# Pooling two batches of v sooner, and spreading the last stage's loads, in a pooled-attention, MLP and mixture-of-experts kernel

## The chip, the cores and the metric

The kernel runs on one core of a Trainium2 chip. The metric is the device time of one execution in microseconds. Before the change three runs took 1186.99, 1190.72 and 1192.93 us, so the median is 1190.72 us.

## The reference

```python
k_p = k.reshape(B, H, Sp, pool, D).mean(axis=3)      # B = H = 8, S = 576, D = 64, pool = 8
v_p = v.reshape(B, H, Sp, pool, D).mean(axis=3)
attn = softmax(scale * q @ k_p.T)
x = (attn @ v_p)  -> (4608, 512)
h = (x @ w1) * (x @ w2) @ w3
y = h @ w_out                                        # d_ff = 1024
logits = y @ w_gate + modality_bias[modality_id]     # 8 experts, top 1
out = gate * (relu(y[mask] @ e_w1[e]) @ e_w2[e])     # per expert
```

Everything is float32. The kernel gets that precision from reduced-precision matmuls by splitting each operand into a high and a low part (`xh` and `xl`, `wh` and `wl`) and running three matmuls for one product: the lines 726, 727 and 728, all in the helper `split`.

## The kernel before, in words

The work falls into a weight stage, nine stages for attention and the first MLP product, a stretch for the second product and the routing, and a loop over expert tiles. Each engine has one instruction queue written out by hand. The engines meet only at semaphores, and an instruction that waits holds up everything behind it on its engine. The same holds for the queues of DMA instructions: SyncE (SP) issues the loads of k, v, x and the weights, ScalarE (ACT) those of q and all stores of `g_rows`.

**Stages.** Stage b (0 to 7) multiplies 512 tokens of batch b by w1 and w2. The 64 tokens of each batch that are left over are collected in DRAM (`left_x`) and make stage 8. A stage has four positions i (`first_position` for stage 0, `position` for the others), and a position has seven products n. Products (`product(b, i, n)`, 12 matmuls each) are the seven block products of a Strassen-like scheme. They rotate through three PSUM banks, shown as `ab`, `x2p` and `rt`. VectorE (DVE) and ACT take them out: `copy_p` (L1139) on ACT and `chain` (L1512) on DVE, which `u2`, `u3`, `u4_c22` and `c12` call in this order in each position. A product may start only once the one three before it has been taken out. At the end of a position GpSimd (POOL) multiplies the two halves: `first_quarter` (L613, L621) and `other_quarters` (L627, L633) write `gst`, and ACT stores that to `g_rows` (`store_g`, L1145, L1148, L1150). L633 may overwrite `gst` only when the stores of the position before have landed (`g_out[1]`), and `u2` of the next position waits for L633.

**Attention for the next batch** is laced into the stage before. `score(b, m)` (L805, m = 0 to 4) are the five rounds of q times pooled k for batch b, all in one pair of PSUM banks `sct`. So each round waits for `sub_done`, which `soft_max` on DVE (L1459, L1461) gives once it has read the round before. `exp_p`, `norm`, `soft_sum` and `soft_turn` finish a round; `exp_p` also issues the q load (`qt`) for the round two later. `weigh_v(b, 0)` and `weigh_v(b, 1)` (L826) multiply the probabilities by pooled v (`vp4`). Then `raw_x`, `x_sum` (L1498), `hi_x` (L1128) and `lo_x` (L1504) make `xf`, `xh` and `xl` of batch b for its own stage.

**Pooling.** `pool_k(b, m)` (L572, L577) and `pool_v(b, m)` (L584, L587) sum groups of eight rows on POOL, in one of two slots `kv`. v of a batch comes in three parts. SP runs `bring_v(b)` in this order: load v 0, load v 1, store v 0, load v 2, store v 1, store v 2, load k of batch b+1 (both halves), and then `spread_v(b)`, four loads of the stored sums into `vp4`, which need all three stores. `weigh_v(b, 0)` waits for those four.

**Behind the last batch** SP loads the four pieces of `left_x` into `xf`, then the four pieces of `w34_rows` (the product w3 times w_out, 520 KB a piece), then `load_g`, which brings `g_rows` back.

`at = 4 * b + i` counts the positions through all stages. `prod_done[n]` counts how often product n has been done.

Of the kernel before, what the change touches and what calls it, by code (L numbers as in the profile page):

```python
# [15 lines left out]
B, H, S, D = 8, 8, 576, 64  # L16
# [30 lines left out]
POS = FC // 2  # L47
# [43 lines left out]
def build(nc, q, k, v, moe_w1, moe_w2, moe_w3, moe_w_out, w_out_t, modality_id, w_gate, modality_bias,  # L91
# [7 lines left out]
    with ctx:  # L99
# [40 lines left out]
        before = small("before", [P, P], BF16, 2)  # L140
# [285 lines left out]
        def _(sp):  # L426
# [63 lines left out]
            sp.wait_ge(xl_ready, BLOCKS * B)  # L490
            for part in range(2):
                for th in range(2):
                    sp.dma_start(xf[:, RAW_X[part][th], :, :],
                                 left_x[:, 2 * part:2 * part + 2, HT * th:HT * (th + 1)]).then_inc(left_in, 16)
            sp.wait_ge(pv_done, 2 * B)
            for n in range(KEPT):
                sp.wait_ge(w34_out[n], 16 * len(range(n, 2 * FC, KEPT)))
            for n in range(4):
                sp.dma_start(w34r[:, 2 * n:2 * n + 2, :], w34_rows[:, 2 * n:2 * n + 2, :]).then_inc(w34_in[n], 16)

            def load_g(t):
# [26 lines left out]
            for t in range(NG):  # L528
                b, g = t // G, t % G
# [26 lines left out]
        def _(pool):  # L556
# [23 lines left out]
            def pool_v(b, m):  # L580
                pool.wait_ge(kv_in[m % 2], 16 * (IN_SLOT[m % 2] * b + 2 + m // 2))
                t = kv[:, m % 2, 0:2 * POOL * D].rearrange("p (c s d) -> p c s d", c=2, s=POOL)
                for w in (4, 2):
                    pool.tensor_tensor(t[:, :, 0:w, :], t[:, :, 0:w, :], t[:, :, w:2 * w, :],  # L584
                                       ALU.add).then_inc(pool_done, 1)
                    pool.wait_ge(pool_done, steps.next())
                pool.tensor_tensor(kv[:, m % 2, 2 * POOL * D:].rearrange("p (c d) -> p c d", c=2), t[:, :, 0, :],  # L587
                                   t[:, :, 1, :], ALU.add).then_inc(vp_ready, 1)
# [21 lines left out]
            def first_quarter(at):  # L610

                pool.wait_ge(x_copied, 3 * at + 2)
                pool.tensor_tensor(pair(p2c[:, :, :]), pair(p2c[:, :, :]), pair(kb[:, 0, :, :]),  # L613
                                   ALU.add).then_inc(p_sums, 1)
                pool.wait_ge(p_sums, 2 * at + 1)
                if at:
                    pool.wait_ge(g_out[0], 16 * at)
                else:
                    for n in (1, 2, 3):
                        pool.wait_ge(w34_out[n], 16 * len(range(n, 2 * FC, KEPT)))  # L620
                pool.tensor_tensor(gst[:, 0, :], p2c[:, 0, :], p2c[:, 1, :], ALU.mult).then_inc(g_ready, 1)  # L621
# [18 lines left out]
            for m in range(2):  # L640
                pool_k(1, m)
            pool_v(1, 0)
            for b in range(STAGES):
                for i in range(POS):
                    first_quarter(POS * b + i)
                    if b == 0 and i < 2:
                        pool_v(1, i + 1)
                    if b and i == 0 and b + 1 < B:
                        pool_v(b + 1, 2)
                    if i == (1 if b else 2) and b + 2 < B:  # L650
                        pool_k(b + 2, 0)
                        pool_k(b + 2, 1)
                    if b and i == 2 and b + 2 < B:
                        pool_v(b + 2, 0)
                    if i == 3 and b + 2 < B:
                        if b == 0:
                            pool_v(2, 0)
                        pool_v(b + 2, 1)
                    other_quarters(POS * b + i)

# [62 lines left out]
        def _(pe):  # L723
# [75 lines left out]
            def score(b, m):  # L799
                may_score(b, m)  # L800
                for n in range(PAIRS):
                    for g in range(4):
                        for a in range(2):
                            rows = slice(D * a, D * (a + 1))
                            mm = pe.matmul(sct[Q * g:Q * (g + 1), a, KEYS * n:KEYS * (n + 1)],  # L805
                                           qt[rows, (AT * b + m) % 2, n, Q * g:Q * (g + 1)], kp[rows, n, :],
                                           start=True, stop=True)
                mm.then_inc(scored, 1)
# [59 lines left out]
                        score(2, 0)  # L868

            def position(b, i):  # L870
                late = 2 if b == 1 and i == 0 else 0
                for n in range(BLOCKS):
                    if i < 2 and n == late and b + 1 < B:
                        score(b + 1, 2 * i + 1)
                    if i < 2 and n == 4 + late and b + 1 < B:
                        score(b + 1, 2 * i + 2)
                    product(b, i, n)
                    if i == 2 and n == 0 and b + 2 < B:
                        score(b + 2, 0)
                    if i == 2 and n == 2 and b + 1 < B:  # L880
                        weigh_v(b + 1, 0)
                    if i == 2 and n == 4 and b + 1 < B:
                        weigh_v(b + 1, 1)
# [543 lines left out]
        def _(dve):  # L1427
# [324 lines left out]
            def position(b, i):  # L1752
                at = POS * b + i
                att = b + 1 < B
                if i == 0:
                    if b > 1:
                        lo_x(b, 6)
                    if att and b > 1:
                        soft_max(b + 1, 1)
                        soft_sum(b + 1, 1)  # L1760
                    u2(at)
                    if b == 1:
                        lo_x(1, 6)
                        soft_sum(2, 0)
                    u3(at)
                    if b == 1:
                        soft_max(2, 1)
                        soft_turn(2, 0)
                    if att and b > 1:
                        soft_max(b + 1, 2)  # L1770
                    u4_c22(at)
                    if b == 1:
                        soft_sum(2, 1)
                        soft_max(2, 2)
                    if att:
                        soft_sum(b + 1, 2)
                        soft_turn(b + 1, 1)
                if i == 1:
                    if att:
                        soft_max(b + 1, 3)  # L1780
                        soft_sum(b + 1, 3)
                        soft_turn(b + 1, 2)
                    u2(at)
                    u3(at)
                    if att:
                        soft_max(b + 1, 4)
                    if b == B:
                        dve.memset(acc[:, :], 0.0).then_inc(dve_done, 1)
                        dve.wait_ge(dve_done, own.next())
                        dve.memset(rb[:, 0, :], 0.0).then_inc(dve_done, 1)  # L1790
                        dve.wait_ge(dve_done, own.next())
                        route_bias(0)
                        lo_w34(0)
                    u4_c22(at)
                    if att:
                        soft_sum(b + 1, 4)
                        soft_turn(b + 1, 3)
                    if b == B:
                        lo_w34(1)
                if i == 2:  # L1800
                    if b + 2 < B:
                        soft_max(b + 2, 0)
                    if att:
                        soft_turn(b + 1, 4)
                    if b + 2 < B:
                        soft_sum(b + 2, 0)
                    u2(at)
                    u3(at)
                    if b == B:
                        lo_w34(2)  # L1810
                    u4_c22(at)
                    if b + 2 < B:
                        soft_turn(b + 2, 0)
                    if b == B:
                        lo_w34(3)
                        lo_g(0)
                    else:
                        x_sum(b + 1, 3)
                if i == 3:
                    if b < B:  # L1820
                        x_sum(b + 1, 4)
                        x_sum(b + 1, 2)
                        lo_x(b + 1, 0)
                        x_sum(b + 1, 5)
                        lo_x(b + 1, 1)
                    u2(at)
                    u3(at)
                    if b < B:
                        lo_x(b + 1, 2)
                    u4_c22(at)  # L1830
                    if b < B:
                        lo_x(b + 1, 3)
                        lo_x(b + 1, 4)
                        lo_x(b + 1, 5)
                    else:
                        lo_g(1)
                c12(at)
# [259 lines left out]
```

## Time and profile before

| | |
|---|---|
| median of three runs | 1190.72 us (1186.99 to 1192.93) |
| the profiled execution | 1193.07 us, span 1191.2 us |
| TensorE (PE) busy | 1158.5 us, 97% of the span |
| PE weight loads busy | 1088.4 us, 91% |
| DVE, ACT, POOL busy | 637.6, 397.6, 400.9 us |
| mean granted TensorE clock | 0.993 of full speed |
| a 256 KB store of `g_rows`, issue to landing, median | 3.2 us |

The span is that of the instructions; 1.9 us lie around it. PE is idle for 32.7 us in all, and only what shortens that idle time or the slow-clock stretches can shorten the run, unless matmuls are taken away.

### The profile page before, as it was taken

To read this page: it belongs to the slowest core of one execution; us is meant where nothing else is said; L and a number is where in the kernel's file an instruction comes from. 1 tells how busy PE (TensorE), PEld (TensorE's weight loads), DVE (VectorE), ACT (ScalarE), POOL (GpSimd) and SP (SyncE) were. 2 spreads that over 40 slices of the span, in tenths; PEclk is the share of its full clock that TensorE was granted. 3 is DMA by queue.
4 is the path that set the end of the run, shared out by engine and by line. 5 is a ranking of instruction groups with operands and counts; after the bars stand their busy time and mean duration, and the time that the engine had idled before them with its cause. 6 is when DMAs were issued, how large, how long until landed. Compare 5 with 4: busy or idle time off the path is not lost.

```text
span 1191.2 us, 29759 instructions
## 1 busy us (share of the span) xinstructions
PE 1158.5 (97%) x12126; PEld 1088.4 (91%) x12127; DVE 637.6 (54%) x1228; ACT 397.6 (33%) x906; POOL 400.9 (34%) x385
## 2 busy tenths in 40 slices
PE   8899889999999999999999999999999999999996
PEld 6789779999999999999999999998998999899895
DVE  0899688798888963653444557622222252222221
ACT  1575355655556541332222324111111141111110
POOL 2337766677766654550000000211211112121111
PEclk9999999999999999999999999999999999999999
DMA  9764363644736314245545555241111101111111
GB/s 348 268 172 140 107 203 83 191 136 133 203 84 193 100 43 159 72 126 140 134 137 132 133 175 176 66 184 44 46 53 35 44 26 55 44 51 46 35 47 41
DMA packets 99890, 137.12 MB, mean 115 GB/s; under 512 B 16835, under 2 KB 66115, under 8 KB 99780
## 3 DMA queue, kind: packets, MB, share of 16 engines
q1 hardware_dynamic: 40340, 78.77, 22.0%
q10 hardware_dynamic: 53040, 36.29, 10.6%
q0 software_dynamic: 6400, 20.50, 5.4%
q8 instruction: 81, 1.33, 0.5%
q14 instruction: 29, 0.24, 0.1%
HBM read 92.99 MB, written 43.06 MB: 114 GB/s over the span
## 4 chain that ended last, share of the span: by engine, by line
PE 55%; DVE 0%; POOL 0%; issue 0%; DMA 0%; ACT 0%; ACTq 0%; POOLq 0%; DVEq 0%
PE ab L727 6%; PE ab L726 6%; PE x2p L726 6%; PE ab L728 6%; PE x2p L728 6%; PE x2p L727 6%; PE rt L727 6%; PE rt L726 6%; PE rt L728 6%; PE sct L917 1%; PE ab L908 0%; DMA out<-y_out,tok_c 0%; DVE gl L1538 0%; POOL gst L633 0%; DVE kb L1512 0%
## 5 line engine op out<-in xcount | busy, mean ns | idle before, releaser
L727 PE MATMUL ab<-xtl,e1h 128*128 128x256 f32 x608 | 170.7, 281 | 0.0
L726 PE MATMUL ab<-xth,e1h 128*128 128x256 f32 x608 | 169.6, 279 | 0.0
L728 PE MATMUL ab<-xth,e1l 128*128 128x256 f32 x608 | 169.3, 278 | 0.0
L1401 ACT ACTIVATE hth<-ab 128x512 fp32r<-128x512 f32 x76 | 45.5, 598 | 333.8 <-PE ab L728 333.8
L706 POOL DMA_INDIRECT out<-y_out,tok_c x38 | 38.4, 1012 | 319.3 <-DVE y_out L2020 318.7
L1999 DVE SCALAR_TENSOR_TENSOR htl<-ab,hth 128x512 fp32r<-128x512 f32 x76 | 52.4, 691 | 156.2 <-ACT hth L1401 156.1
L727 PEld LDWEIGHTS ab<-xtl,e1h 128*128 128x128 f32 x608 | 114.5, 188 | 0.7
L726 PEld LDWEIGHTS ab<-xth,e1h 128*128 128x128 f32 x608 | 114.1, 188 | 1.0 <-issue 0.4
L728 PEld LDWEIGHTS ab<-xth,e1l 128*128 128x128 f32 x608 | 114.3, 188 | 0.0
L726 PE MATMUL x2p<-xh,wh 128*128 128x256 f32 x336 | 98.2, 292 | 5.1 <-DVE kb L1512 4.8
L1086 ACT ACTIVATE pb<-pb,rc 128x72 f32<-128x72 f32 x320 | 83.2, 347 | 59.7 <-DVE rc L1473 59.7
L726 PE MATMUL ab<-xh,wh 128*128 128x256 f32 x336 | 96.8, 288 | 1.9 <-DVE kb L1512 1.4
L726 PE MATMUL rt<-xh,wh 128*128 128x256 f32 x336 | 97.3, 290 | 0.7 <-DVE kb L1512 0.6
L727 PE MATMUL x2p<-xl,wh 128*128 128x256 f32 x336 | 95.4, 284 | 0.0
L727 PE MATMUL rt<-xl,wh 128*128 128x256 f32 x336 | 95.2, 283 | 0.0
L727 PE MATMUL ab<-xl,wh 128*128 128x256 f32 x336 | 94.7, 282 | 0.0
L728 PE MATMUL x2p<-xh,wl 128*128 128x256 f32 x336 | 94.4, 281 | 0.0
L728 PE MATMUL rt<-xh,wl 128*128 128x256 f32 x336 | 94.1, 280 | 0.0
L728 PE MATMUL ab<-xh,wl 128*128 128x256 f32 x336 | 93.7, 279 | 0.0
L1538 DVE TENSOR_TENSOR gl<-gr,gh 128x1024 fp32r<-128x1024 f32 x36 | 45.2, 1256 | 78.4 <-ACT gh L1159 78.4
L633 POOL TENSOR_TENSOR gst<-kb 128x768 f32<-128x768 f32 x36 | 72.2, 2004 | 41.8 <-DVE kb L1512 33.2
L726 PE MATMUL x2p<-w34h,gh 128*128 128x260 f32 x288 | 82.1, 285 | 0.0
(229 smaller groups left out, 3344.8 us busy)
## 6 DMA issues: line engine op xcount, KB each, us to landing
gr<-g_rows SPq DMA_DIRECT2D x36, 512.0 KB, 4.3
kv<-in_v SPq DMA_DIRECT2D x24, 512.0 KB, 4.6
qt<-in_q ACTq DMA_DIRECT2D x38, 256.0 KB, 3.2
kv<-in_k SPq DMA_DIRECT2D x16, 576.0 KB, 5.3
g_rows<-gst ACTq DMA_DIRECT2D x72, 128.0 KB, 2.6
g_rows<-gst ACTq DMA_DIRECT2D x36, 256.0 KB, 3.2
x_rows<-xr SPq DMA_DIRECT2D x36, 256.0 KB, 3.7
stage<-in_moe_w SPq DMA_DIRECT2D x8, 1024.0 KB, 8.5
```

Source lines behind the costliest of these rows:

```text
L633: pool.tensor_tensor(gst[:, 1:4, :], kb[:, 1:4, 0, :], kb[:, 1:4, 1, :], ALU.mult).then_inc(g_ready, 1)
L706: pool.indirect_dma_start(out=out, out_offset=bass.IndirectOffsetOnAxis(ap=tok_c[:, n:n + 1], axis=0), in_=y_out[:, half, :], in_offset=No ...
L726: pe.matmul(outp, lh, rh, start=first, stop=False)
L727: pe.matmul(outp, lh, rl, start=False, stop=False)
L728: return pe.matmul(outp, ll, rh, start=False, stop=last)
L917: mm = pe.transpose(bank[:, n, :], xg[:, 2 * r + half, n * P:(n + 1) * P], ident[:, :])
L1086: ins = act.activation(p, p, ACT.Copy, scale=rc[r % 2][:, h:h + 1])
L1401: act.activation(hth[:, 2 * n:2 * n + 2, :].rearrange("p f n -> p (f n)"), ab[n // 2][:, n % 2, :], ACT.Relu).then_inc(hth_ready, 1)
L1538: dve.tensor_tensor(gl[t % RING][:, :, :], gr[t % RING][:, :, :], gh[t % RING][:, :, :].bitcast(F32), ALU.subtract).then_inc(gl_ready, 1)
L1999: dve.scalar_tensor_tensor(out=htl[:, fs, :].rearrange("p f n -> p (f n)"), in0=ab[n // 2][:, n % 2, :], scalar=0.0, in1=hth[:, fs, :].rea ...
```

## The change

No instruction of a computing engine is added or taken away. Five things are moved or given a wait:

- POOL pools v part 1 of batch 1 before stage 0 instead of in its first position, and part 2 in the first position instead of the second.
- POOL pools v part 0 of batch 2 before `first_quarter` of stage 0's fourth position, where it stood behind it.
- PE: `score(2, 1)` in stage 1's first position stands before product 3, where it stood before product 2. (`score(2, 2)` stays before product 6.)
- DVE: `soft_turn(2, 0)` stands behind `u4_c22`, where it stood ahead of it.
- SP: the four `left_x` loads wait one after the other for products 0, 2, 4 and 6 of position 28 (stage 7's first), and the four `w34_rows` loads for product 2 of positions 29, 30, 31 and 32.

```diff
@@ SP, behind the last batch
             for part in range(2):
                 for th in range(2):
+                    sp.wait_ge(prod_done[4 * part + 2 * th], POS * (B - 1) + 1)
                     sp.dma_start(xf[:, RAW_X[part][th], :, :],
                                  left_x[:, 2 * part:2 * part + 2, HT * th:HT * (th + 1)]).then_inc(left_in, 16)
...
             for n in range(4):
+                sp.wait_ge(prod_done[2], POS * (B - 1) + 2 + n)
                 sp.dma_start(w34r[:, 2 * n:2 * n + 2, :], w34_rows[:, 2 * n:2 * n + 2, :]).then_inc(w34_in[n], 16)
@@ POOL
             pool_v(1, 0)
+            pool_v(1, 1)
             for b in range(STAGES):
                 for i in range(POS):
+                    if b == 0 and i == 3:
+                        pool_v(2, 0)
                     first_quarter(POS * b + i)
-                    if b == 0 and i < 2:
-                        pool_v(1, i + 1)
-                    if b and i == 0 and b + 1 < B:
+                    if i == 0 and b + 1 < B:
                         pool_v(b + 1, 2)
...
                     if i == 3 and b + 2 < B:
-                        if b == 0:
-                            pool_v(2, 0)
                         pool_v(b + 2, 1)
@@ PE, position
-                late = 2 if b == 1 and i == 0 else 0
+                before = (3, 6) if b == 1 and i == 0 else (0, 4)
                 for n in range(BLOCKS):
-                    if i < 2 and n == late and b + 1 < B:
-                        score(b + 1, 2 * i + 1)
-                    if i < 2 and n == 4 + late and b + 1 < B:
-                        score(b + 1, 2 * i + 2)
+                    if i < 2 and n in before and b + 1 < B:
+                        score(b + 1, 2 * i + 1 + before.index(n))
                     product(b, i, n)
@@ DVE, position, i == 0
                     if b == 1:
                         soft_max(2, 1)
-                        soft_turn(2, 0)
...
                     u4_c22(at)
                     if b == 1:
+                        soft_turn(2, 0)
                         soft_sum(2, 1)
                         soft_max(2, 2)
```

The files differ by one or two line numbers, so `pool_v` is L584 and L587 before and L586 and L589 after the change.

POOL from the last part of `pool_v(1, 0)` to `other_quarters` of position 1, before the change:

```order
41 L587 TENSOR_TENSOR kv<-kv 128x128
42 L613 TENSOR_TENSOR p2c<-p2c,kb 128x512
43 L621 TENSOR_TENSOR gst<-p2c 128x256
44 L584 TENSOR_TENSOR kv<-kv 128x2x256
45 L584 TENSOR_TENSOR kv<-kv 128x2x128
46 L587 TENSOR_TENSOR kv<-kv 128x128
47 L627 TENSOR_TENSOR kb<-kb 128x512
48 L633 TENSOR_TENSOR gst<-kb 128x768
49 L613 TENSOR_TENSOR p2c<-p2c,kb 128x512
50 L621 TENSOR_TENSOR gst<-p2c 128x256
51 L584 TENSOR_TENSOR kv<-kv 128x2x256
```

The same place after it:

```order
41 L589 TENSOR_TENSOR kv<-kv 128x128
42 L586 TENSOR_TENSOR kv<-kv 128x2x256
43 L586 TENSOR_TENSOR kv<-kv 128x2x128
44 L589 TENSOR_TENSOR kv<-kv 128x128
45 L615 TENSOR_TENSOR p2c<-p2c,kb 128x512
46 L623 TENSOR_TENSOR gst<-p2c 128x256
47 L586 TENSOR_TENSOR kv<-kv 128x2x256
48 L586 TENSOR_TENSOR kv<-kv 128x2x128
49 L589 TENSOR_TENSOR kv<-kv 128x128
50 L629 TENSOR_TENSOR kb<-kb 128x512
```

Rows 42 to 44 are now part 1 of batch 1's v, ahead of `first_quarter` of position 0, and rows 47 to 49 are part 2, which began at row 51.

SP behind the last `spread_v`, with the semaphores that each load waits for, before the change:

```order
74 L493 DMA xf<-left_x 128x2x256 [waits xl_ready,tl_out]
75 L493 DMA xf<-left_x 128x2x256 x3
76 L499 DMA w34r<-w_rows 128x1040 [waits w34_out3,w34_out2,w34_out4,w34_out1,w34_out5,w34_out0,pv_done]
77 L499 DMA w34r<-w_rows 128x1040 x3
78 L510 DMA gr_111<-g_rows 128x1024 [waits g_out1,g_out0,xl_ready]
```

The same place after it:

```order
74 L494 DMA xf<-left_x 128x2x256 [waits prod_done0,xl_ready,tl_out]
75 L494 DMA xf<-left_x 128x2x256 [waits prod_done2]
76 L494 DMA xf<-left_x 128x2x256 [waits prod_done4]
77 L494 DMA xf<-left_x 128x2x256 [waits prod_done6]
78 L501 DMA w34r<-w_rows 128x1040 [waits w34_out3,w34_out4,w34_out2,w34_out5,w34_out1,prod_done2,w34_out0,pv_done]
79 L501 DMA w34r<-w_rows 128x1040 [waits prod_done2] x3
80 L512 DMA gr_111<-g_rows 128x1024 [waits g_out1,g_out0,xl_ready]
```

The eight loads keep their order; each of the last seven has a wait of its own, and the loads of `g_rows` stand behind them as before.

## Rows read from the trace of the kernel before

**Rows 1.** The list of PE's waits: us in total, times, longest.

```profile
PE sct L805 <- DVE pb L1461: 6.6, 3, 3.5
PE x2p L726 <- DVE kb L1512: 4.8, 6, 2.2
```

**Rows 2.** Timeline of PE, start of `weigh_v(1, 0)`: start, duration, what, idle before.

```profile
122.13 0.37 PE L826 MATMUL ab<-ptt,vp 32*64 32x144 f32 x6 [2.48 <-DMA vp<-v_rows]
```

**Rows 3.** Timeline of SP in stage 0.

```profile
95.13 12.66 SPq L443 DMA_DIRECT2D v_rows<-kv  x2
110.22 0.81 SPq L430 DMA_DIRECT2D kv<-in_k  x2
111.21 2.03 SPq L451 DMA_DIRECT2D vp<-v_rows  x4
```

**Rows 4.** Timeline of POOL in stage 0.

```profile
89.42 1.29 POOL L613 TENSOR_TENSOR p2c<-p2c,kb 128x512 f32<-128x512 f32 x1 [11.94 <-ACT p2c L1139]
...
92.47 2.10 POOL L584 TENSOR_TENSOR kv<-kv 128x512 f32<-128x512 f32 x2
94.64 0.46 POOL L587 TENSOR_TENSOR kv<-kv 128x128 f32<-128x128 f32 x1
...
122.94 1.84 POOL L633 TENSOR_TENSOR gst<-kb 128x768 f32<-128x768 f32 x1
...
135.56 0.79 POOL L587 TENSOR_TENSOR kv<-kv 128x128 f32<-128x128 f32 x1
```

**Rows 5.** Timeline of DVE, stage 0 and the start of stage 1.

```profile
83.12 0.69 DVE L1504 TENSOR_TENSOR xl<-xf,xh 128x512 fp32r<-128x512 f32 x1
...
130.35 0.69 DVE L1512 TENSOR_TENSOR kb<-rt,kb 128x512 f32<-128x512 f32 x1 [9.97 <-PE rt L728]
130.96 1.83 DVE L1498 TENSOR_TENSOR xf<-xf 128x512 f32<-128x512 f32 x2
...
133.31 1.58 DVE L1504 TENSOR_TENSOR xl<-xf,xh 128x512 fp32r<-128x512 f32 x1
134.81 1.22 DVE L1498 TENSOR_TENSOR xf<-xf 128x512 f32<-128x512 f32 x1
...
141.51 0.68 DVE L1512 TENSOR_TENSOR kb<-ab,kb 128x512 f32<-128x512 f32 x1
...
150.64 0.76 DVE L1461 TENSOR_TENSOR pb<-sct,mx 128x576 f32<-128x576 f32 x1
```

**Rows 6.** Timeline of PE: `score(2, 1)` and `score(2, 2)` in position 4.

```profile
141.70 0.87 PE L805 MATMUL sct<-kp,qt 64*32 64x72 f32 x64 [1.21 <-issue]
...
151.54 1.25 PE L805 MATMUL sct<-kp,qt 64*32 64x72 f32 x64 [2.39 <-DVE pb L1461]
```

**Rows 7.** Busy time and granted clock behind that wait.

```profile
152.00:155.00 3.00, 3.00 (x64) 2.80 (x44) 2.93 (x7) 0.52 (x3) 0.00 (x0) 0.51 0.87 241
```

**Rows 8.** Timeline of SP, the loads behind the last batch.

```profile
445.34 1.92 SPq L493 DMA_DIRECT2D xf<-left_x  x4
447.50 3.45 SPq L499 DMA_DIRECT2D w34r<-w_rows  x4
```

**Rows 9.** The two `g_rows` stores issued at 447.00 and 447.40, to landing.

```profile
DMA to landing us min/median/max: 5.5/8.3/11.1
```

**Rows 10.** Timeline of POOL, `other_quarters` of position 28.

```profile
458.66 1.81 POOL L633 TENSOR_TENSOR gst<-kb 128x768 f32<-128x768 f32 x1 [5.98 <-DMA g_rows<-gst]
```

**Rows 11.** Timeline of PE, first matmuls of products before and behind the wait.

```profile
457.52 0.28 PE L726 MATMUL ab<-xh,wh 128*128 128x256 f32 x1
...
465.76 0.28 PE L726 MATMUL ab<-xh,wh 128*128 128x256 f32 x1
...
467.20 0.28 PE L726 MATMUL x2p<-xh,wh 128*128 128x256 f32 x1
```

**Rows 12.** The q load issued at 112.14, beside k and `vp4` loads, to landing.

```profile
DMA to landing us min/median/max: 8.5/8.5/8.5
```

**Rows 13.** Timeline of PE, `score(1, 4)`.

```profile
108.50 0.88 PE L805 MATMUL sct<-kp,qt 64*32 64x72 f32 x64
```

## The prediction, made before the changed kernel ran

> **What bounds the kernel now.** The page gives PE as 97% busy, and no edit takes a matmul away. It can pay only where PE waits or runs slowly, so I first read the list of PE's waits [rows 1]. The longest entries are waits for `soft_max` to free the score banks (6.6 us in three waits, one of them in the weight stage, which the change doesn't touch) and for a `chain` operation on DVE (4.8 us in six waits, one alone 2.2 us). A third is a wait for a DMA: `weigh_v(1, 0)` stood 2.48 us for `vp4` [rows 2]. Then I followed each wait back through the timelines of SP, POOL and DVE.
>
> **Edit 1, v of batch 1 sooner.** `spread_v(1)` was issued at 111.21, because it needs the third store of pooled v. The two stores in the first SP row ended at 95.13 + 12.66 = 107.79: the one at 95.13 is part 1, the other part 2 [rows 3]. POOL had made part 1 by 94.64 + 0.46 = 95.10, only behind `first_quarter(0)`, for which it had sat idle for 11.94 us until 89.42 [rows 4]. Now part 1 fills that idle time and part 2 takes part 1's old place. So the third store goes out at 95.13 instead of about 107.46 (107.79 less the 0.33 of an issue): 12.3 us sooner. k of batch 2 goes from 110.22 to about 97.9, and the spread from 111.21 to about 98.9. PE got the spread at 122.13 [rows 2], 10.9 us after its first issue. Now it is there at about 110, and PE wants it at 122.13 - 2.48 = 119.65. The wait goes, with 10 us to spare: **2.5 us**. Next in line for `weigh_v(1, 0)` is the probability of round 4, turned on DVE before DVE fell idle for 9.97 us at 120.4 (130.35 - 9.97) [rows 5], and that is the end of the operation behind it. So nothing new stops PE there.
>
> Does the rest follow? DVE's idle time before 130.35 ended with PE's product `rt` [rows 5]. DVE is then busy almost to 151.4, and `score(2, 2)` waits for the end of that run, 150.64 + 0.76 = 151.40 [rows 5, 6]. So the chain that sets the pace starts from a PE product, and moves forward by the whole 2.5 us. Later stages wait only for semaphores, so they move too.
>
> **Edit 2, v part 0 of batch 2 ahead of `first_quarter(3)`.** POOL is free at 122.94 + 1.84 = 124.78 [rows 4]. One `pool_v` lasts 2.6 us, from 92.47 to 95.10 [rows 4], so it ends at 127.4. `first_quarter(3)` ends some 2.1 us later, at 129.5, where ACT needs it for `store_g` at about 131.3 - 2.5 = 128.8. Next behind that store on ACT is `hi_x(1, 2)`, whose input DVE makes only at 134.81 + 1.22 - 2.5 = 133.5 [rows 5]: no cost. POOL's pooling ended at 135.56 + 0.79 = 136.35 [rows 4], 6.0 us behind DVE's start at 130.35. Now it ends at about 127.4 + 2.1 + 2.7 = 132.2, 4.4 us behind DVE's new start at 127.8. That matters because DVE is slower beside POOL. A `lo_x` takes 0.69 us alone and 1.58 at 133.31. Two `x_sum` took 1.83 and one took 1.22 where 0.69 each would do [rows 5]. Together that is 0.45 + 0.89 + 0.53 = 1.9 us, the most that the edit can give. Zero is the least. POOL covers a quarter less of that stretch (4.4 against 6.0 us), so I take a quarter, **0.5 us**.
>
> The Trainium skill (SBUF — State Buffer, Who interferes with whom) says that a VectorE operation with two SBUF inputs and a GpSimd operation that reads SBUF exclude each other for the whole of an instruction. The slower rows above agree with it in kind. By that rule `pool_v(1, 1)` now also stands against DVE's `lo_w` run before stage 0, and in full it would add its 2.6 us to it. The trace before has a margin there: `lo_x(0, 1)`, which the second product needs, ends at 83.12 + 0.69 = 83.8 [rows 5], and the copy of that product reaches POOL only at 89.42 [rows 4], where a product takes 1.4 us. I put the cost at 0, with 0.5 us as its bound.
>
> **Edit 3, `score(2, 1)` one product later.** PE stood 1.21 us before it [rows 6]. The page names no engine, but `score(2, 1)` needs `sub_done` of `soft_max(2, 0)`, which DVE ends just before 141.51. Product 2, which now goes first, needs `c12` of position 3, and that is the DVE operation at 141.51 to 142.19 [rows 5]. So PE waits for DVE all the same, 0.5 us longer, does the product first, and the score after it. Product 3 then starts later by about 0.7 us. But `score(2, 2)` waits at 151.54 for DVE's run to end, after 2.39 us of idling [rows 6]. That idling absorbs 0.7 us either way. Price: **0**, bounds -0.2 (PE's clock is spared) and +0.3.
>
> **Edit 4, `soft_turn(2, 0)` behind `u4_c22`.** Both stand between `soft_max(2, 1)` and `soft_max(2, 2)`, which frees the banks for `score(2, 3)`. The sum between the two is the same. It saves at most the 0.1 us for which DVE stood for `norm(2, 0)`. **0**.
>
> **Edit 5, the loads behind the last batch.** Before, 1 MB of `left_x` was issued from 445.34 and 2.1 MB of `w34_rows` from 447.50 to 450.95 [rows 8]. Two `g_rows` stores were issued in that crowd and took up to 11.1 us to land [rows 9], where the page's median is 3.2. POOL stood 5.98 us for them until 458.66 [rows 10], `u2` of position 29 stood for POOL, and PE for `u2`: that is the 2.2 us of the second entry [rows 1]. From 457.52 to 465.76 PE did three products in 8.24 us. The pitch at full clock is 467.20 - 465.76 = 1.44 us [rows 11], so 8.24 - 3 x 1.44 = **3.9 us** are lost: the wait and a stretch at half clock behind it.
>
> After the change only two or three `left_x` pieces (256 KB each, 2.8 us apart) are in flight beside these stores. The first `w34_rows` piece waits for the product that ended 1.2 us before 457.52, about 456.3. Even at 5.5 us to landing, the faster of the two [rows 9], the stores are there by 452.9, when POOL (458.66 - 5.98 = 452.7) wants them. POOL then needs 1.81 us, so `gst` is done by 454.7, and `u2` needs it only when its own product is done at 456.3. The 3.9 us go in full. Each `w34_rows` piece now meets the stores of one position alone. The pieces land by about 461, 471, 481 and 491, and their splits start after 500, so nothing waits. `load_g` of tile 0 stands behind the last piece and goes from 489.8 to about 487.8, as all has moved by 3.9: also no later. The spread costs nothing.
>
> The Trainium skill (DMA: Bandwidth & Descriptors, Queues, rings and completion order) says that a DMA's semaphore lands only after every earlier write of the same DMA engine, across queues. By that rule even a single 520 KB piece holds up a store issued behind it. The trace has no single piece beside a store, so I weigh it as a rival.
>
> **The sum.** 2.5 + 0.5 + 0 + 0 + 3.9 = 6.9 us. The profiled execution took 1193.07 us, so its like would take 1186.2. That execution was 2.35 us above the median of 1190.72, and 1190.72 - 6.9 = **1183.8 us**. A measurement of this kernel tells a change from none at about 0.5%, which is 6.0 us: the forecast lies just beyond it.
>
> **Rivals.**
>
> - *The clock comes back too.* Behind the wait at 151.54 the clock fell to half (0.51 from 152 to 155) [rows 7]. The score took 1.25 us where others take 0.87, and the product behind it some 1.0 us more than its like: 1.4 us. Behind the 2.48 us wait for `vp4` it did not fall. With other idle times before it, the fall may stay away: 6.9 + 1.4 = 8.3, 1182.4 us. Against it: the 2.4 us wait itself stays. Chance 0.13.
> - *The first gain is lost.* k and `vp4` loads now run from 98 to about 108 and meet the q load for `score(1, 4)`, issued at about 101. One in the same crowd took 8.5 us to land [rows 12]. That gives 109.6, and PE wants it at 108.50 [rows 13]: up to 1.1 us on PE directly, and a fall of the clock behind it another 1.4. For it: the crowd is the same. Against it: the q load now goes 3.2 us behind the k loads, not 1.9, and fewer stores are among them. With this and no gain from edit 2, 2.5 + 3.9 - 2.5 = 3.9: 1186.8 us. Chance 0.13.
> - *The late loads don't do what they should.* The first piece or the `left_x` pieces still hold the stores beyond 456 us, and only the early part pays: 3.0 us, 1187.7. Chance 0.08.
> - *Slower: each piece makes its own wait.* If one 520 KB piece alone holds the stores of its position for over 7.5 us (issued at about 455.5, wanted at about 463), the single wait becomes four. Four at 3.9 us are 15.6 against 3.9 before, less 3.0 of the early part: 8.7 us slower, 1199.4. Against it: six times the bytes cost 11.1 us, so one piece should cost some 3. Chance 0.03.
>
> The forecast keeps 0.63.
>
> **How the numbers follow.** The forecast's own range is the bounds of its terms (2.5, with 0 to 1.9 for edit 2, 3.9, and 0.5 either way for edits 1 and 3) and the scatter of the runs before (1186.99 to 1192.93, so some 2 us on a median): 1181 to 1187 us. With the clock and the lost first gain, 8 times in 10 it is 1179.5 to 1188.0. The line for faster by over 0.5% is 1184.77 us. The forecast is below it in about six of ten cases (0.38), the first rival in nearly all (0.12), the others in few (0.02): 0.52 faster. The slower case has 0.03, and 0.45 is left for no change that could be told.
>
> **What would show it.** In the trace of the changed kernel: `spread_v(1)` near 99 us, and no wait before L826 near 119.6. `pool_v(2, 0)` ends near 127.4, and DVE's chain starts near 127.8. PE still waits about 2.4 us for `soft_max(2, 1)`, near 148.5. POOL's L633 of position 28 starts within 0.5 us of 452.9 less the early gain, and no PE wait over 1 us lies between 450 and 500 us. It would be wrong if `score(1, 4)` waits for q, if a store of `g_rows` beside a `w34_rows` piece takes over 7.5 us, or if the wait before `score(2, 2)` grows by as much as the early gain.

## The result and the profile after

| | before | changed |
|---|---|---|
| median of 20 runs | 1192.98 us | 1187.56 us |
| lowest to highest | 1186.99 to 1196.44 | 1186.21 to 1192.96 |
| ratio, 95% interval | 1 | 0.9961 (0.9949 to 0.9973) |
| profiled execution, its span | 1193.07, 1191.2 us | 1191.04, 1189.3 us |

The change makes the kernel 0.39% faster. That is 4.65 us of 1190.72, where 6.9 were forecast, and within the half per cent that was called no change. The profiled execution of the changed kernel was one of its longer ones, so the pair of traces shows only 2.0 us between them.

First the list of PE's waits in the changed kernel (us in total, times, longest), against [rows 1]:

```profile
PE sct L806 <- DVE pb L1460: 9.2, 3, 5.0
PE ab L727 <- DVE kb L1511: 2.9, 4, 1.9
PE x2p L727 <- DVE kb L1511: 2.4, 6, 0.9
PE sct L806 <- DMA qt<-in_q: 0.6, 1, 0.6
PE ab L727 <- DVE xl L1503: 0.5, 1, 0.5
PE rt L727 <- DVE xl L1503: 0.4, 1, 0.4
```

The 2.2 us in the entry for `x2p` are gone. Waits for a q load (0.6 us) and for `xl` are new: the two for `xl` shown here and a third of 0.3 us make 1.2 us. Of the 9.2 us, 5.0 lie in the weight stage, which the change doesn't touch. SP and PE next (timelines: start, duration, what, idle before):

```profile
84.32 14.53 SPq L443 DMA_DIRECT2D v_rows<-kv  x2
100.08 0.81 SPq L430 DMA_DIRECT2D kv<-in_k  x2
101.06 3.17 SPq L451 DMA_DIRECT2D vp<-v_rows  x4
```

```profile
83.94 0.89 PE L806 MATMUL sct<-kp,qt 64*32 64x72 f32 x64
85.33 0.39 PE L727 MATMUL ab<-xh,wh 128*128 128x256 f32 x1 [0.51 <-DVE xl L1503]
...
93.68 0.88 PE L806 MATMUL sct<-kp,qt 64*32 64x72 f32 x64 [1.26 <-issue]
...
112.60 0.89 PE L806 MATMUL sct<-kp,qt 64*32 64x72 f32 x64 [0.64 <-DMA qt<-in_q]
...
123.47 0.36 PE L827 MATMUL ab<-ptt,vp 32*64 32x144 f32 x6
...
152.69 0.87 PE L806 MATMUL sct<-kp,qt 64*32 64x72 f32 x64 [2.29 <-DVE pb L1460]
...
157.08 0.88 PE L806 MATMUL sct<-kp,qt 64*32 64x72 f32 x64 [1.91 <-DVE pb L1460]
```

`weigh_v(1, 0)` at 123.47 has no idle time before it: the 2.48 us of [rows 2] are gone. Yet it starts 1.34 us later than before. Follow the scores up to it. `score(1, 0)` stood at 83.42 before and at 83.94 now. `score(1, 1)` stood at 90.28 and now stands at 93.68. So the stretch between the two grew from 6.86 to 9.74 us, by 2.9, and that ate the whole wait. DVE shows why. First the kernel before, then the changed one:

```profile
73.90 6.93 DVE L1449 TENSOR_TENSOR wl<-wr,wh 128x1024 fp32r<-128x1024 f32 x5
...
89.42 0.76 DVE L1461 TENSOR_TENSOR pb<-sct,mx 128x576 f32<-128x576 f32 x1
```

```profile
74.74 9.23 DVE L1448 TENSOR_TENSOR wl<-wr,wh 128x1024 fp32r<-128x1024 f32 x5
...
92.82 0.76 DVE L1460 TENSOR_TENSOR pb<-sct,mx 128x576 f32<-128x576 f32 x1
```

The run of five `lo_w` before stage 0 takes 2.3 us longer. The second row of each is the subtraction of `soft_max(1, 0)`, which gives the score banks back to PE. It ended at 90.18 before, and `score(1, 1)` started at 90.28. It ends at 93.58 now, and the score starts at 93.68. PE started 0.1 us behind it both times, and in twelve of the thirteen profiled executions of this document. So a delay of DVE here is a delay of PE, though the row of the changed kernel says "issue". POOL, which works beside DVE there, in the changed kernel:

```profile
77.70 1.32 POOL L589 TENSOR_TENSOR kv<-kv 128x128 f32<-128x128 f32 x1
78.98 3.92 POOL L586 TENSOR_TENSOR kv<-kv 128x512 f32<-128x512 f32 x2
82.97 1.32 POOL L589 TENSOR_TENSOR kv<-kv 128x128 f32<-128x128 f32 x1
...
454.95 1.85 POOL L635 TENSOR_TENSOR gst<-kb 128x768 f32<-128x768 f32 x1 [0.24 <-DVE kb L1511]
```

The rows at 78.98 and 82.97 are `pool_v(1, 1)`: 5.3 us beside the `lo_w` run, where the same two rows took 2.10 and 0.46 by themselves [rows 4]. The last row is `other_quarters` of position 28. Its 5.98 us for a `g_rows` store [rows 10] have gone. SP there, and the stores issued between 440 and 460 us, to landing:

```profile
447.23 7.30 SPq L494 DMA_DIRECT2D xf<-left_x  x4
458.56 31.07 SPq L501 DMA_DIRECT2D w34r<-w_rows  x4
```

```profile
DMA to landing us min/median/max: 1.8/2.6/4.0
```

### The profile page after: what moved, and what is told of

Same layout as the page of the kernel before. It is cut to its first block, busy times and chain, and to the rows that moved or that the text cites. A ratio compares the mean times of both kernels' runs of the same rounds, so it can differ in the third digit from the quotient of the medians.

```text
span 1189.3 us, 29760 instructions
## 1 busy us (share of the span) xinstructions
PE 1154.7 (97%) x12126; PEld 1083.7 (91%) x12127; DVE 641.3 (54%) x1228; ACT 397.3 (33%) x906; POOL 404.3 (34%) x385
## 3 DMA queue, kind: packets, MB, share of 16 engines
q10 hardware_dynamic: 53040, 36.29, 10.8%
## 4 chain that ended last, share of the span: by engine, by line
PE 55%; DVE 0%; POOL 0%; issue 0%; DMA 0%; ACT 0%; ACTq 0%; POOLq 0%; DVEq 0%
PE ab L728 6%; PE x2p L727 6%; PE ab L727 6%; PE ab L729 6%; PE x2p L729 6%; PE x2p L728 6%; PE rt L728 6%; PE rt L727 6%; PE rt L729 6%; PE sct L916 1%; PE ab L907 0%; DMA out<-y_out,tok_c 0%; DVE gl L1537 0%; POOL gst L635 0%; DVE kb L1511 0%
```

## The experiments

The port theory: POOL's additions slow DVE's `lo_w` run, the run's end sets `soft_max(1, 0)`, and that sets `score(1, 1)`. So the early part costs nearly what it gives, and what is left is the late part. The rivals: the early part gives its gain and the late part doesn't; or the stretch grows for a reason other than POOL's work beside the run. In all diffs the first lines are those of the kernel named.

**Edit 5 by itself** (the kernel before, plus this):

```diff
+                    sp.wait_ge(prod_done[4 * part + 2 * th], POS * (B - 1) + 1)
                     sp.dma_start(xf[:, RAW_X[part][th], :, :],
...
+                sp.wait_ge(prod_done[2], POS * (B - 1) + 2 + n)
                 sp.dma_start(w34r[:, 2 * n:2 * n + 2, :], ...
```

> The kernel before with edit 5 alone (the eight loads behind the last batch each wait for a product). Port theory (the late edit pays its 3.9 us in full, and the early edits together pay almost nothing, because v part 1 of batch 1 is now pooled beside VectorE's lo_w run): 3.9 us faster, ratio 0.9967. Rival (the early edits pay 3 us as forecast and the late edit pays only the rest of the 4.7 us measured, because it moves a wait elsewhere): 1.7 us faster, ratio 0.9986. In the profile both expect no wait of PE over 1 us between 440 and 500 us.

Measured: 0.9975 (0.9960 to 0.9990), so 3.0 us. Both expected values lie in that interval, so the time alone doesn't choose between them. The wait for `vp4` is there, at 3.3 us, as the edit doesn't touch it.

**The change without edit 5** (the two lines above taken out):

> The changed kernel without edit 5. Port theory: within 1 us of the kernel before, ratio 0.999 to 1.000; the lo_w run of five before stage 0 takes about 9 us where it took 6.9, and PE's first product of stage 0 waits for lo_x. Rival (early edits pay 3 us): ratio 0.9975.

Measured: 0.9984 (0.9969 to 0.9999), so 1.9 us. The `lo_w` run took 7.89 us, the stretch between the scores 9.89, and `weigh_v(1, 0)` had no wait. The time again fits both sides: it lies between them, and the interval reaches both. The two parts add up to 4.9, against 4.65 for both. The run is shorter than expected because `pool_v(1, 1)` began only 1.1 us before its end; it slowed the DVE operations behind the run instead. PE in position 28 shows what edit 5 takes away there, at a smaller size than before:

```profile
459.75 0.39 PE L725 MATMUL x2p<-xh,wh 128*128 128x256 f32 x1 [1.97 <-DVE kb L1509]
```

**`pool_v(1, 1)` before the stages, and nothing else** (the kernel before, part 2 at its old place):

```diff
             pool_v(1, 0)
+            pool_v(1, 1)
...
-                    if b == 0 and i < 2:
-                        pool_v(1, i + 1)
+                    if b == 0 and i == 1:
+                        pool_v(1, 2)
```

> The kernel before with one thing moved: v part 1 of batch 1 is pooled before stage 0; part 2 stays in the second position, so that vp4 is as late as before. It has the suspected cost and none of the gain. Port theory: slower by the 1.5 to 2.5 us that VectorE loses to POOL before stage 0, less what the old wait for vp4 (2.5 us, near 120) takes up, because a DMA that is not later absorbs a late PE: so between 0 and 1 us slower in total, ratio 1.000 to 1.001, but with the wait before weigh_v(1, 0) shrunk from 2.5 to below 1 us and the waits for lo_x in position 0 there. Rival: no waits for lo_x in position 0, the wait before weigh_v(1, 0) stays 2.5 us, ratio 1.000.

Measured: 1.0011 (0.9991 to 1.0030). The `lo_w` run took 8.67 us, the stretch 9.58, and `weigh_v(1, 0)` still waited 1.75 us for `vp4`, more than I had expected: part 2 is the third store, and it stayed late. By itself the step makes the stretch longer and brings no gain. In the time nothing can be told.

**Both parts in position 0** (the changed kernel, with `pool_v(1, 1)` moved behind `first_quarter(0)`, ahead of part 2):

```diff
             pool_v(1, 0)
-            pool_v(1, 1)
...
                     first_quarter(POS * b + i)
+                    if b == 0 and i == 0:
+                        pool_v(1, 1)
```

> The changed kernel, but v part 1 of batch 1 is pooled behind first_quarter of position 0, and part 2 directly behind it. Nothing is pooled beside the lo_w run any more, and vp4 should still be there near 112 us, before PE wants it near 119.6. Port theory: this gives what the forecast gave, 6.4 to 6.9 us faster than the kernel before, ratio 0.9942 to 0.9946, and 2 us faster than the changed kernel. Rival (the port costs nothing, the start of the run scatters by itself): as the changed kernel, ratio 0.996.

Measured: 0.9932 (0.9907 to 0.9957), in six runs. The run took 7.06 us, the stretch 6.98, and `weigh_v(1, 0)` had no wait at 118.25. Here the gain of edit 1 came without its cost. The same kernel again, beside the changed one on one chip:

> The kernel with both parts of v of batch 1 pooled in position 0, once more. Port theory: 2 to 3 us faster than the changed kernel on the same chip, ratio to the kernel before 0.993 to 0.9945. Rival (the first time was a lucky chip): ratio as the changed kernel, 0.996.

> The changed kernel once more, to stand on the same chip as the next two. Port theory and start-scatter rival alike: ratio 0.996. What tells them apart is the trace: by the port theory the stretch from score(1, 0) to score(1, 1) is again 9.5 to 9.9 us, where kernels without v part 1 beside the lo_w run have 6.9 to 7.9; by the rival it falls back to about 7.

Measured: 0.9955 (0.9940 to 0.9971) for this version and 0.9973 (0.9962 to 0.9984) for the changed kernel, so 1.9 us between the medians, with intervals that overlap. The rival's 0.996 is not excluded by this. In this execution of the first, POOL was late: the end of `pool_k` and all of `pool_v(1, 0)` lay beside the run, which took 8.81 us, and the stretch 8.50. In that of the changed kernel the run took 8.55 and the stretch 8.74, where 9.5 to 9.9 were expected. So this pair of traces doesn't separate the two kernels. Over all executions they do differ: with `pool_v(1, 1)` ahead of the stages the stretch took 8.74 to 9.89 us (four executions, mean 9.49), and with it in position 0 and nothing else of POOL's added or held back, 6.65 to 8.50 (six, mean 7.30). That is 2.2 us on average, where the first pair of traces shows 2.9.

**The same, without edits 2 to 4** (the kernel before, plus edit 5, and `pool_v(1, 1)` and `(1, 2)` both behind `first_quarter(0)`):

> The kernel before with both parts of v of batch 1 pooled behind first_quarter of position 0 and with edit 5, but without edits 2, 3 and 4 (v of batch 2, the later score round, the later soft_turn). By the forecast's terms edit 2 is worth 0.5 us and the others nothing, so this should be 0.5 us slower than both_again, ratio 0.994 to 0.995. Rival: in the traces so far the stretch from weigh_v(1, 0) to score(2, 3) shrank from 34.0 to 33.6 us with those edits, so they are worth 0.4 us by sum; either way under 1 us.

Measured: 0.9962 (0.9947 to 0.9978), a little slower than expected. In this execution POOL had ended `pool_v(1, 0)` before the run, and did nothing beside it. DVE, then POOL, then PE:

```profile
73.02 5.72 DVE L1452 TENSOR_TENSOR wl<-wr,wh 128x1024 fp32r<-128x1024 f32 x5
...
87.90 0.76 DVE L1464 TENSOR_TENSOR pb<-sct,mx 128x576 f32<-128x576 f32 x1
```

```profile
71.39 1.32 POOL L589 TENSOR_TENSOR kv<-kv 128x128 f32<-128x128 f32 x1
```

```profile
88.86 0.89 PE L808 MATMUL sct<-kp,qt 64*32 64x72 f32 x64
```

5.72 us is the length of the run with nothing beside it: even the kernel before paid 1.2 us for `pool_v(1, 0)`. PE starts 0.2 us behind the end of the subtraction (88.66), the only one of the thirteen that shows any room there.

**Extra additions** (the kernel before, and on POOL, ahead of the stages, a write and three additions on a tile that is free there; `pool_v(1, 1)` stays at its old place; a wait on ACT for the last addition is not shown; it stands where the addition is long done):

```diff
             pool_v(1, 0)
+            pool.memset(pair(p2c[:, :, :]), 0.0).then_inc(extra_done, 1)
+            for n in range(3):
+                pool.wait_ge(extra_done, n + 1)
+                pool.tensor_tensor(pair(p2c[:, :, :]), pair(p2c[:, :, :]), pair(p2c[:, :, :]),
+                                   ALU.add).then_inc(extra_done, 1)
```

> The kernel before, with three additions of 128x512 on a buffer that nothing else uses at that time added to POOL between the pooling of v part 0 of batch 1 and stage 0, beside VectorE's run of five lo_w. Nothing is taken away. Port theory: the run of five takes 8.5 to 9.5 us instead of 6.9 to 7.6, though no data and no semaphore of it hang on POOL, and score(1, 0) to score(1, 1) takes over 9 us. Rival (in the changed kernel VectorE was late for another reason, as later w1 and w2 parts or a late probability): 6.9 to 7.6 us.

DVE, POOL and PE of that run:

```profile
71.97 9.23 DVE L1457 TENSOR_TENSOR wl<-wr,wh 128x1024 fp32r<-128x1024 f32 x5
```

```profile
76.11 0.52 POOL L644 MEMSET p2c<- 128x512 f32 x1
76.71 5.39 POOL L647 TENSOR_TENSOR p2c<-p2c 128x512 f32<-128x512 f32 x3
```

```profile
91.48 0.88 PE L811 MATMUL sct<-kp,qt 64*32 64x72 f32 x64 [1.20 <-issue]
```

Work that has nothing to do with v makes the run 9.23 us long and the stretch between the scores 10.32. So it is POOL's additions beside DVE, not the loads or stores of v. This is one execution, and what it shows is the trace, not a time. Both engines pay: an addition took 1.80 us here (5.39 / 3), where a 128x512 operation took 1.29 (the first row of [rows 4]).

**Extra writes** (the same place, seven writes of zeros in place of the additions), to see if it is POOL's reads that count:

> The kernel before, with seven writes of zeros to a free SBUF tile on POOL (128 x 512 each, no operand read) where the run of extra adds had a memset and three adds; nothing waits for them but the second copy of a product on ACT, some 10 us later. The DVE run of five lo_w is the measure: 5.7 us by itself, 6.9 to 7.6 beside one pool_v, 9.2 beside the three adds. Contention by reads alone (what POOL reads from SBUF holds DVE up): the sets add nothing, 6.9 to 7.6 us beside the one pool_v. Contention by any access of POOL: 8.5 us and more. Score(1, 0) to score(1, 1) follows it: 6.9 to 7.9 us by the first, 8.7 to 10.3 by the second.

For the run nothing follows. POOL was late in this execution, and the writes started at 82.38, when the run had ended at 79.60. What lay beside the run were POOL's additions for k and v of batch 1, and it took 8.13 us, the stretch 8.18. But the writes lay beside the DVE operations behind the run. POOL, then DVE:

```profile
81.65 0.78 POOL L588 TENSOR_TENSOR kv<-kv 128x128 f32<-128x128 f32 x1
82.38 4.02 POOL L647 MEMSET p2c<- 128x512 f32 x7
```

```profile
82.05 1.66 DVE L1505 TENSOR_TENSOR xf<-xf 128x512 f32<-128x512 f32 x2
83.63 0.68 DVE L1511 TENSOR_TENSOR xl<-xf,xh 128x512 fp32r<-128x512 f32 x1
84.23 1.41 DVE L1505 TENSOR_TENSOR xf<-xf 128x512 f32<-128x512 f32 x2
```

The first row still met the end of `pool_v(1, 0)`. The other two lay wholly beside writes and took 0.68 and 1.41 us, as long as in the kernel before at 83.12 and 83.72 (0.69 and 1.41), where POOL did nothing. So writes of this size didn't slow them, where additions do. This is one execution.

**All of v behind the run** (the version with both parts in position 0, and also `pool_v(1, 0)` held back):

```diff
+            pool.wait_ge(wl_ready, BLOCKS + 6)
             pool_v(1, 0)
```

> The changed kernel, with pool_v(1, 0) held on POOL until DVE has done the run of five lo_w before stage 0, and pool_v(1, 1) and (1, 2) behind first_quarter(0). Port theory: the run of five lo_w takes 5.7 to 6.0 us whatever the timing of the start, score(1, 0) to score(1, 1) 6.6 to 6.9 us, and the spread loads of v still leave before 103 us, so V(1, 0) has no wait over 0.5 us; the ratio is 0.992 to 0.996, at or below that of the version with only (1, 1) and (1, 2) moved (0.9932 and 0.9955 in two measurements). If the length of that stretch hung on something else than POOL's work beside it, it stays at 6.9 us or more and the ratio at that of the changed kernel, 0.9961 to 0.9973.

Measured: 0.9961 (0.9944 to 0.9979). DVE, then POOL:

```profile
75.39 5.72 DVE L1450 TENSOR_TENSOR wl<-wr,wh 128x1024 fp32r<-128x1024 f32 x5
81.03 0.17 DVE L1672 CAST mod<-mod_raw 128x36 f32<-128x36 int32 x1
81.23 1.26 DVE L1674 TENSOR_SCALAR mod<-mod 128x36 f32<-128x36 f32 x1
82.53 0.69 DVE L1505 TENSOR_TENSOR xl<-xf,xh 128x512 fp32r<-128x512 f32 x1
83.14 2.08 DVE L1499 TENSOR_TENSOR xf<-xf 128x512 f32<-128x512 f32 x2
```

```profile
81.19 2.62 POOL L586 TENSOR_TENSOR kv<-kv 128x512 f32<-128x512 f32 x2 [8.63 <-DVE wl L1450]
```

The run is 5.72 us long, as expected. But the stretch took 7.38 us, not 6.6 to 6.9, and the ratio is no better than that of the changed kernel. The additions now lie beside the operations behind the run: the one on `mod` took 1.26 us (0.18 in the changed kernel), and two `x_sum` 2.08 (1.41 there). The collision was moved, not removed, and the chain to `soft_max(1, 0)` runs through these operations too. In the trace this version is as fast as those with both parts in position 0 (see the sum below), so why its ratio isn't stays open.

**The w34 half of edit 5 by itself** (edit 5 alone, without the first of its two waits, so that `left_x` is issued at once):

> The kernel before with only the second half of edit 5: the four w34_rows pieces are issued one position apart, the left_x pieces at once as before. If the 2.1 MB of w34_rows were what held the g_rows stores, the run has nearly all that edit 5 alone gave: the wait of POOL before L633 of position 28 gone or under 1 us, the stores landing in 5 us or less, ratio 0.9975 as measured for edit 5 alone, within 0.9960 to 0.9990. If the four left_x pieces at once (1 MB) hold the stores as well, POOL waits 2 us or more, stores take 6 us or more, and the ratio is 0.9990 or above.

Measured: 0.9976 (0.9963 to 0.9990), as much as the whole of edit 5. SP, and the stores between 440 and 460 us to landing:

```profile
443.75 1.92 SPq L493 DMA_DIRECT2D xf<-left_x  x4
454.79 30.68 SPq L500 DMA_DIRECT2D w34r<-w_rows  x4
```

```profile
DMA to landing us min/median/max: 1.9/3.3/5.2
```

POOL waited at most 0.8 us for a store, and PE had no wait over 0.3 us from 440 to 472 us. So the 2.1 MB of `w34_rows` were the crowd that mattered. Beside the 1 MB of `left_x` alone a store took up to 5.2 us, and nobody waited for it.

## Why the prediction was right and wrong

The forecast was 1183.8 us and the median came out at 1187.56, 3.8 us above it. Some of that isn't the change: the 20 runs of the kernel before have their median at 1192.98, 2.3 us above the three that the forecast started from. The rest is the gain, which fell short of 6.9 us.

**The step that failed: `pool_v(1, 1)` beside the `lo_w` run.** "I put the cost at 0, with 0.5 us as its bound." It cost 2.3 to 2.9 us in the profiled pair (the run alone, and the stretch between the scores), and 2.2 us of that stretch on average over the executions. The rule of the Trainium skill (SBUF — State Buffer, Who interferes with whom), which I had quoted and worked out at 2.6 us, was the better guide: the `lo_w` run went from 6.93 to 9.23 us. It isn't a full exclusion here, though. The run and the two `pool_v` take 5.72 and 5.2 us alone, 10.9 one after the other, and both were done in 9.6 (74.68 to 84.29). The contention was known, and the error was in the margin. I looked at two users of DVE's work, `lo_x(0, 1)` and the copy of product 2, and found over 5 us of room. The one that mattered stood further on in DVE's queue, from 88.63: `soft_max(1, 0)`, which frees the banks for `score(1, 1)`, 0.1 us before PE took them. The PE row has no idle time in front of it, which looks like room. It was a tie.

**Edit 1's gain: right in mechanism, the size only a lower end.** Predicted: spread near 99, no wait. Measured: 101.06 for the spread (the whole is 2.9 us late by then), and the 2.48 us gone. I left it at that because the clock did not fall behind this wait in the trace that I had. In others it does. This is the kernel with the w34 half of edit 5, where PE waited 2.13 us for `vp4` until 119.60, and behind it the kernel before, where it waited 2.48 until 122.13 (the last three columns: granted clock, DMA share, GB/s):

```profile
122.00:125.00 3.00, 3.00 (x18) 3.00 (x18) 0.00 (x0) 1.61 (x6) 0.81 (x1) 0.61 0.19 72
```

```profile
122.00:125.00 3.00, 2.87 (x106) 2.71 (x107) 0.00 (x0) 1.05 (x6) 2.64 (x2) 1.00 0.65 196
```

Six profiled executions keep this wait. Behind 2.13, 2.45 and 3.33 us the clock fell, and `weigh_v(1, 0)` to `score(2, 0)` took 12.4 us. Behind 1.61, 1.75 and 2.48 us, and in all seven executions without the wait, it took 10.8 to 11.0. The 1.5 us carry on to `score(2, 2)` (31.0 against 29.1 to 29.5). So where nothing is added to POOL's work beside the run, the wait that edit 1 removes was worth 2.5, 3.6, 4.0 and 4.8 us in the four executions that show it, 3.7 on average.

With `pool_v(1, 1)` moved to position 0, three measurements gave 0.9932, 0.9955 and, without edits 2 to 4, 0.9962, against 0.9961 and 0.9973 for the changed kernel. The means differ by 0.0017, or 2.0 us, close to the 2.2 us of the stretch. But the intervals overlap, and the version with all of v behind the run gave 0.9961. So the collision and its way to PE are shown in the traces. That it costs 2 us of the whole time is likely, and not shown beyond the noise.

**Edit 2: half of it, within its bounds.** Edits 2 and 3 act on one stretch, and edit 3 was put at nothing. The three DVE operations that POOL slows took 4.63 us before (1.83, 1.58 and 1.22 in [rows 5]) and take 4.36 now. From `weigh_v(1, 0)` to `score(2, 2)` it took 29.41 us before and 29.22 now. Where the clock stayed up, the other kernels with edits 2 to 4 took 29.11 to 29.41, and those without 29.42 to 29.51. So some 0.2 us, where I took 0.5.

**Edit 3: 0, as put. Edit 4: 0.2 where 0 was put.** PE waits for `c12` ahead of product 2, by 1.91 us for 1.21, and the wait before `score(2, 2)` absorbs it (2.29 for 2.39). `score(2, 2)` to `score(2, 3)`, the stretch of edit 4, takes 4.38 or 4.39 us in all six executions with it and 4.59 or 4.60 in all seven without. DVE sets its length: it no longer stands 0.1 us for `norm(2, 0)` before `soft_turn(2, 0)`, which I had as the most. The other 0.1 stays open.

**Edit 5: right in mechanism, the size depends.** Before, the loss from 457.52 to 465.76 was 3.9 us, and all of it is gone in the changed kernel. By itself the edit measured 3.0 us (1.2 to 4.8). The five executions that keep the old loads show why: PE's wait was 2.29, 2.21, 1.97, 1.71 and 1.43 us. Behind 2.21 and 1.97 the clock fell; two products took 4.5 us where 2.9 is usual. Behind the other three it did not, the longest among them. The loss, reckoned as in the prediction, was 3.9 and 3.8 us with the fall and 2.6, 2.0 and 1.7 without, 2.8 on average. I had priced one execution with a fall as if all had it, the reverse of the error in edit 1.

**Rivals.** The q load did come late, as the second said: `score(1, 4)` waited 0.64 us. In the other six executions with v sooner it waited 0.45 and 0.26 us in two, and not at all in four. The rival had up to 1.1. That was small against the collision. The clock of the first rival did come back. The same window as in [rows 7] now reads:

```profile
152.00:155.00 3.00, 2.31 (x76) 2.20 (x76) 3.00 (x5) 1.26 (x4) 0.00 (x0) 1.00 0.47 123
```

But it gave nothing, not 1.4 us, since PE waits for DVE at the end of the stretch in any case: 1.91 us now, 0.73 before. The second execution of the changed kernel shows it, where the clock did fall (0.51 from 149 to 152):

```profile
148.56 1.25 PE L806 MATMUL sct<-kp,qt 64*32 64x72 f32 x64 [2.31 <-DVE pb L1460]
...
152.94 0.87 PE L806 MATMUL sct<-kp,qt 64*32 64x72 f32 x64 [0.56 <-DVE pb L1460]
```

The stretch takes 4.38 us with the fall and 4.39 without. The kernel with `pool_v(1, 1)` moved alone, which lacks edit 4, takes 4.59 at a granted clock of 1.00, as the kernel before does at 0.51. The price of the first rival was time that PE spends waiting anyway.

The last rival did not occur, though a single piece does hold a store. A 256 KB store issued 0.7 us ahead of one piece took 6.2 us to land, in the second execution with both parts in position 0, where I had reckoned with some 3. In the changed kernel the stores beside the last piece and the first load of `g_rows` took 5.4 to 6.0 us. POOL waited 0.9 us for one of them, and PE not over 0.3.

The sum again, for the profiled pair: 2.5 to 4.0 for the wait, less 2.3 for the collision and 0.6 for q, 0.2 each for edits 2 and 4, and 3.0 for edit 5. That makes 3.0 to 4.5 us, beside 4.65 from the ratio (3.2 to 6.1).

One stretch holds the waits that edits 1 to 4 touch, so it measures them together, clock and all: from `score(1, 0)` to `score(2, 3)`.

| kernels | executions | from `score(1, 0)` to `score(2, 3)`, us | mean |
|---|---|---|---|
| early part as before | 4 | 72.7, 73.8, 75.4, 75.9 | 74.4 |
| early part as changed | 3 | 71.5, 73.1, 73.3 | 72.6 |
| both parts in position 0 (70.2 without edits 2 to 4) | 3 | 69.9, 70.2, 71.9 | 70.7 |
| all of v behind the run | 1 | 70.8 | |

(The run with extra writes is counted with the first row, as its writes lay behind the run.) So the early part gave 1.8 us, beside 1.9 measured, and 1.9 more were to be had. With the 2.8 of edit 5 that makes 4.6, beside 4.65. Each row has few executions, and they scatter by up to 3.2 us, so the close fit is in part luck.

## What to carry to other kernels

Work filled into an idle stretch of one engine is not free if another engine works on SBUF beside it: price it on that engine, and follow that engine's queue to everything it owes, not only to the next two users. A wait's price is not complete without the clock behind it, and one trace shows only one of its two outcomes. A slow clock costs nothing where the engine waits for another at the end of the stretch. A matmul without idle time in front may be tied with its releaser: compare the end of the releaser's operation with the start of the matmul before calling it room. A large load whose data is wanted much later should not be issued whole beside small stores that somebody waits for.

## What the runs showed of the hardware

- The five 128x1024 subtractions on DVE take 5.72 us alone, 6.9 to 7.6 beside one pooling of v on POOL, 7.9 to 8.8 where a late pooling of k lay beside them too, and 8.6 to 9.2 beside two poolings of v, or beside one and three extra additions. POOL is slowed as well: an extra addition took 1.80 us, where an operation of that size takes 1.29, and a `pool_v` goes from 2.6 to 5.3. Writes of zeros on POOL left DVE's operations as long as they are alone.
- Whether the clock falls behind a wait isn't told by its length alone: at `vp4` it fell behind 2.13 and 2.45 us and not behind 2.48, and in position 28 behind 1.97 and 2.21 and not behind 2.29. At these places a fall costs 1.5 us. Where DVE sets the pace, as from `score(2, 2)` to `score(2, 3)`, it costs nothing (4.38 us for 4.39).
- Around the last batch the pitch of a product was 1.40 us in some stretches and 1.44 in others of the same trace, with a granted clock of 1.00 in both. Both kernels show both, and most switches came at a short wait of PE. I don't know why. It makes up to 0.3 us in the stretches compared here.
